# A product with two weights side by side, and the place of the scores of wide tiles

## The reference

```python
for t in range(S):                                   # S = 768, heads of D = 40
    y[:, :, t] = np.einsum('bhd,bhde->bhe', rt, state)
    Sa = np.einsum('bhde,bhe->bhd', state, at)
    state_decay = state * wt[:, :, None, :] - np.einsum('bhd,bhe->bhde', Sa, bt)
    state = state_decay + np.einsum('bhd,bhe->bhde', vt, kt)
...
h = np.maximum(x @ w_in, 0.0)                        # 320 -> 1024
conv_out += conv_w[k][None, None, :] * hp[:, k:k + S, :]
return (h * gate @ w_out).astype(np.float32)
...
for e in range(E):                                   # E = 4, Hd = 64
    scores = scale * (q @ k.transpose(0, 2, 1))
    scores = np.where(causal, -1000000000.0, scores)
    scores = scores - scores.max(-1, keepdims=True)
    a = np.exp(scores)
    a /= a.sum(-1, keepdims=True) + 1e-09
    ye = a @ v @ wo[e]
```

## Time and profile before

| | us |
|---|---|
| three runs | 920.96, 911.47, 918.24 (median 918.24) |
| the profiled execution | 923.58 |
| its span, first to last instruction | 921.9 |
| PE busy | 824.6 (89%), 11,872 matmuls |
| weight loads | 597.0 (65%) |
| DVE busy | 559.7 (61%) |
| ACT busy | 317.4 (34%) |
| POOL busy | 259.5 (28%) |
| mean granted clock of PE | 0.946 |

### The profile page before, as it was taken

One profiled execution on the slowest core, in us unless ns is written; L12 is line 12 of the kernel. 1 busy time (PEld: TensorE's weight loads), 2 busy tenths in 40 slices (PEclk: granted clock), 3 DMA queues, 4 the chain that ended last, 5 costly groups with the idle time before them and its releaser, 6 DMA issues.

```text
span 921.9 us, 27713 instructions
## 1 busy us (share of the span) xinstructions
PE 824.6 (89%) x11872; PEld 597.0 (65%) x11872; DVE 559.7 (61%) x1235; ACT 317.4 (34%) x741; POOL 259.5 (28%) x525
## 2 busy tenths in 40 slices
PE   3428989998999988889998999988999998999988
PEld 3428889988998988864465654545644656545555
DVE  8995795878599742136528645357464277354474
ACT  4102331323133232222227542246432266322364
POOL 2087777778778877000000000000000000000000
PEclk9999895979599798899999999999999979999999
DMA  3645575657566574620100000100001000000000
GB/s 117 153 85 122 126 163 113 134 139 140 122 157 138 113 158 102 157 78 26 44 1 15 16 15 1 43 0 23 15 8 43 1 8 22 16 1 0 1 15 30
DMA packets 130922, 61.33 MB, mean 67 GB/s; under 512 B 106544, under 2 KB 119792, under 8 KB 130800
## 3 DMA queue, kind: packets, MB, share of 16 engines
q1 hardware_dynamic: 96156, 32.61, 16.3%
q10 hardware_dynamic: 34644, 26.95, 11.3%
HBM read 45.37 MB, written 14.16 MB: 65 GB/s over the span
## 4 chain that ended last, share of the span: by engine, by line
PE 75%; DVE 11%; issue 5%; ACT 5%; POOL 2%; DMA 1%; SPq 0%; ACTq 0%; DVEq 0%
PE ps_all L808 8%; PE ps_all L792 8%; PE ps_scan L105 5%; PE ps_all L852 5%; PE ps_scan L188 4%; PE ps_all L918 4%; PE ps_all L900 4%; PE ps_all L930 4%; PE ps_scan L130 3%; PE ps_scan L167 3%; PE ps_all L795 3%; PE ps_all L802 2%; PE ps_all L835 2%; PE ps_scan L122 2%; PE ps_scan L114 2%
## 5 line engine op out<-in xcount | busy, mean ns | idle before, releaser
L328 POOL TENSOR_TENSOR t_update<-solver_then_w_down 128x133 f32<-128x133 f32 (+13 forms) x251 | 118.6, 473 | 88.1 <-DMA solver_then_w_down<-l_blocks 39.1
L330 POOL TENSOR_TENSOR solver_then_w_down<-solver_then_w_down,t_update 128x133 f32<-128x133 f32 (+13 forms) x251 | 132.7, 529 | 19.7
L105 PE MATMUL ps_scan<-decayed_a_and_eye,scaled_then_x 40*128 40x104 f32 x768 | 67.6, 345 | 46.5 <-DVE decayed_a_and_eye L362 45.2
L1129 DVE TENSOR_REDUCE minus_max<-ps_all 128x1 f32<-128x128 f32 (+5 forms) x96 | 55.3, 617 | 66.8 <-PE ps_all L904 66.8
L105 PEld LDWEIGHTS ps_scan<-decayed_a_and_eye,scaled_then_x 40*128 40x128 f32 x768 | 62.8, 252 | 48.6 <-issue 47.7
L808 PE MATMUL ps_all<-gated,solver_then_w_down 128*128 128x384 f32 x256 | 91.1, 499 | 0.0
L792 PE MATMUL ps_all<-scaled_then_x,inputs_then_w_up 128*128 128x384 f32 x256 | 88.8, 490 | 1.8 <-ACT ak_l_then_ffn L970 1.8
L1028 ACT ACTIVATE probs_t<-ps_all 128x512 f32<-128x512 f32 (+3 forms) x128 | 55.1, 452 | 69.9 <-PE ps_all L918 69.3
L808 PEld LDWEIGHTS ps_all<-gated,solver_then_w_down 128*128 128x128 f32 x256 | 46.0, 189 | 44.6 <-issue 19.1
L792 PEld LDWEIGHTS ps_all<-scaled_then_x,inputs_then_w_up 128*128 128x128 f32 x256 | 47.6, 190 | 36.3 <-ACT ak_l_then_ffn L970 6.0
L232 ACT ACTIVATE x_rhs<-ps_scan 128x320 f32<-128x320 f32 x48 | 21.0, 438 | 141.3 <-PE ps_scan L122 70.5
(11 more groups left out here) (117 smaller groups left out, 1523.8 us busy)
## 6 DMA issues: line engine op xcount, KB each, us to landing
r_t_and_v_t<-in_rv ACTq DMA_DIRECT2D x48, 160.0 KB
inputs_then_w_up<-in_x ACTq DMA_DIRECT2D x46, 160.0 KB
solver_then_w_down<-l_blocks SPq DMA_DIRECT2D x22, 256.0 KB, 4.6
uv_and_ruv<-in_v ACTq DMA_DIRECT2D x48, 80.0 KB, 3.7
y_t<-y_out SPq DMA_DIRECT2D x24, 160.0 KB
out<-out_rows SPq DMA_DIRECT2D x24, 160.0 KB, 1.8
inputs_then_w_up<-in_x ACTq DMA_DIRECT2D x46, 81.4 KB
inputs_then_w_up<-in_x ACTq DMA_DIRECT2D x46, 80.0 KB
```

The costliest lines, as they stand in the source:

```text
L105: last = nc.tensor.matmul(PS[:, o:o + ROWS], weights, AL[c % NK][rows(h), p, :], start=True, stop=True)
L328: return (lambda: eng.tensor_tensor(tmp[:, 0:cols, 0:rest], l[:, s:s + 1, s + 1:BLK].broadcast_to(shape), t[:, 0:cols, s:s + 1].broadcast_ ...
L330: lambda: eng.tensor_tensor(t[:, 0:cols, s + 1:BLK], t[:, 0:cols, s + 1:BLK], tmp[:, 0:cols, 0:rest], ALU.subtract))
L1129: nc.vector.tensor_reduce(NM[:, v:v + 1], PS[:, first_bank(v) * 512:first_bank(v) * 512 + n], AX.X, ALU.min).then_inc(m["nm"], 1)
```

## The change

Two edits.

First, the tiles of r, v and u become one, `v_t_u_t_r_t` (`VUR`, three buffers): for each position p three pieces of 64 columns. For head 0 they are v, u, r, for head 1 they are r, u, v, so that v and u (or u and v) stand side by side and make one weight operand of 40 x 128. `uv_r` then has one product for each p and h, 16 in all, that writes all 128 partitions of `PH[h]`. ACT copies u into the middle piece, and `u_t` goes. The DRAM input has the same three pieces, the middle one zero, and the DMA loads all three.

```diff
-    RV = [sb(f"r_t_and_v_t{n}", [ROWS, 2, P8, C]) for n in range(3)]
-    RT = [RV[n][:, 0, :, :] for n in range(3)]
-    VT = [RV[n][:, 1, :, :] for n in range(3)]
+    VUR = [sb(f"v_t_u_t_r_t{n}", [ROWS, P8, 3, C]) for n in range(3)]
+    RT = lambda n, h: VUR[n][rows(h), :, 2 - 2 * h, :]
+    UT = [VUR[n][:, :, 1, :] for n in range(3)]
...
                 for h in range(2):
-                    nc.tensor.matmul(PH[h][own(h), seg(p, C)], VT[n % 3][rows(h), p, :], RT[n % 3][rows(h), p, :],
-                                     start=True, stop=True)
-                for h in range(2):
-                    last = nc.tensor.matmul(PH[h][own(1 - h), seg(p, C)], UT[rows(h), p, :], RT[n % 3][rows(h), p, :],
+                    last = nc.tensor.matmul(PH[h][:, seg(p, C)], VUR[n % 3][rows(h), p, h:h + 2, :].rearrange("r k t -> r (k t)"), RT(n % 3, h)[:, p, :],
                                             start=True, stop=True)
...
-                act.dma_start(RV[n % 3][rows(h), :, :, :].rearrange("r k p t -> r (k p t)"),
-                              in_rv[n, h].rearrange("r k p t -> r (k p t)")).then_inc(m[f"r{n % 3}"], 16)
+                act.dma_start(VUR[n % 3][rows(h), :, :, :].rearrange("r p k t -> r (p k t)"),
+                              in_rv[n, h].rearrange("r p k t -> r (p k t)")).then_inc(m[f"r{n % 3}"], 16)
...
-                nc.scalar.activation(UT[:, :, :], by8(PU, C)[0:ROWS], ACT.Copy, scale=-1.0).then_inc(m["ut_sb"], 1)
+                nc.scalar.activation(UT[n % 3], by8(PU, C)[0:ROWS], ACT.Copy, scale=-1.0).then_inc(m["ut_sb"], 1)
```

Second, in PE's loop over pairs, `scores(w)` of a wide pair moves behind the transposes of unit 2(w-2) and `values(w-3)`:

```diff
         for w in range(NW + LAG_O - 1):
-            if w < NW:
+            wide = 2 * w >= WIDE
+            if w < NW and not wide:
                 scores(w)
             if 0 <= w - LAG_T < NW:
                 transposes(2 * (w - LAG_T))
             if 0 <= w - LAG_PV < NW:
                 values(w - LAG_PV)
+            if w < NW and wide:
+                scores(w)
             if 0 <= w - LAG_T < NW:
                 transposes(2 * (w - LAG_T) + 1)
```

More of the change, by code:

```diff
@@ L61, in recurrence @@
     ZS = sb("x_rhs2", [128, P8, D])
-    UT = sb("u_t", [ROWS, P8, C])
     ST = [sb(f"state{x}", [ROWS, P8, D]) for x in range(NPAR)]
@@ L176, in out_from_state @@
                     o = place(6, p) + D
-                    nc.tensor.matmul(PS[rows(h), o:o + C], STT[n % 2][rows(h), p, :], RT[n % 3][rows(h), p, :],
+                    nc.tensor.matmul(PS[rows(h), o:o + C], STT[n % 2][rows(h), p, :], RT(n % 3, h)[:, p, :],
                                      start=(p % 4 == 0), stop=False, skip_group_check=True)
```

6 lines of the change are left out of this document (5 added, 1 removed).

## The result

The changed kernel took **986.92 us** as a median of four runs (982.8 to 994.74), the kernel before 919.6 us beside it (911.47 to 922.18): ratio 1.076 (1.066 to 1.086). Slower was right, but the time lies 31 us above the forecast of 956 and outside its range of 938 to 976. The profiled execution took 988.72 us, 65.1 more than that of before; its recurrence ends 31.5 us later (435.7 instead of 404.2), and what comes behind it takes 33.6 us more, 8.4 for each of the four batches.

The account below looks back on a forecast made before the run. PE was taken to bound the recurrence, and a loop over other engines the wide attention pairs. Change 1 (+18 us) and change 2 (+20) made +38: 961.6 us profiled, 956 us as a median, range 938 to 976.

Parts of the forecast that it names:

- What bounds the kernel: Recurrence bound by PE, 28% of the time at the low clock; wide attention pairs by a loop over DVE and ACT.
- Change 1, the block: uv_r in the recurrence: weight loads set the pace, 2.0 us high and 3.7 low against 1.0 and 1.9; +27.5 us.
- Change 1, the holes: Ten PE waits for "issue" before x_from_state (L122) in the recurrence vanish, with matmul tails: -8.9 us.
- Change 1, the clock: Recurrence: low share kept as before, 4.4 of 24 steps low; no added cost in the sum.
- Layout, loads and the strided copy: Recurrence: loads growing from 160 to 240 KB and u's copy in 8 pieces are hidden; priced at nothing.
- Change 2: Attention, pairs 8 to 11: scores behind transposes and values join a longer loop over DVE; 5 us a batch, +20 us.
- upper bound: Attention: PE's idle stretches of 1 to 2.5 us also bring a low-clock window, some 3 us more a batch.
- hidden weights: Rival, uv_r: only streaming counts, the block stays at 1.0 us and the holes close; 929 us, chance 0.07.
- the instruction count: Rival, uv_r: instruction count alone sets the pace, the block takes 0.5 us; 917 us, no change, chance 0.02.
- the fit into the wait: Rival, attention: transposes and values fit into the wait for exponentials, scores(9) starting by 507.9; 926 us, chance 0.05.
- both at once: Rival: uv_r's weights hidden and transposes and values fitting into the wait; -19 us, 899 us, chance 0.03.
- the clock rival: Two more low-clock stretches in the recurrence or one in every attention: +12 to +20 us, 968 to 976, chance 0.13.

Follow-up runs that it names:

- e1: Kernel before with only the new v, u, r layout and uv_r in 16 products, attention order unchanged; 941.59 us, 26.8 over before.
- e11: The edits of e3 and e7 in one kernel; median of four runs 928.48 us, ratio 1.010 to before; fastest run 912.95 us, ratio 0.994.
- e3: e1 with each of uv_r's 16 products streaming r twice, 128 columns, the second 64 never read; 918.91 us, 22.7 less than e1.
- e4: Kernel before with the new tile, its 240 KB loads and strided copy of u, but uv_r in 32 products; 925.23 us, ratio 1.012.
- e6: Kernel before with only the values of three pairs earlier ahead of the wide scores, transposes behind; 957.87 us, 41.3 over before, ratio 1.047.
- e9: e6 with DVE's copy of o_t moved ahead of the maxima for wide pairs; 934.58 us, ratio 1.020 to the kernel before.
- e2: Kernel before with only the wide pairs' order changed: scores of pairs 8 to 11 behind transposes and values; 956.19 us, 41.4 over before.
- e8: Kernel before with the 32 products of uv_r issued twice over; 983.38 us, ratio 1.075.
- e7: Kernel before with x_from_v, x_from_state, first_blocks and all_blocks streaming 64 columns instead of 40, the extra 24 unread; 914.61 us, ratio 0.999.

## Why the prediction was wrong, step by step

The forecast added 38 us, the change cost 67.3. The step that failed is the clock, which the sum put at nothing in both parts; the holes and the waits of part 2 were mis-sized.

**What bounds the kernel.** Right: the recurrence by PE, the wide pairs by a loop over other engines. It did not ask what keeps the clock up, and this is where it failed.

**Change 1, the block: right.** Priced at 2.0 us high and 3.7 low against 1.0 and 1.9, +27.5 in all. Measured 1.93 us high; low it is 91.30 - 87.69 = 3.61 in e1. e11 has one with 128 columns streamed wholly at the low level, 3.71 us from its start to the next one by PE's timeline:

```profile
226.95 3.78 PE L160 MATMUL ps_scan<-v_t_u_t_r_t 40*128 40x128 f32 x32 [2.53 <-issue]
230.66 0.58 PE L125 MATMUL ps_scan<-state,decayed_a_and_eye 40*64 40x64 f32 x6
```

The rest of the recurrence grew by 18.6 us in the changed kernel and 20.7 in e1, with the low time taken out; 23 blocks of 0.93 us more are 21. The Trainium skill, "TensorE: Matmul & The Clock Gate", section "LDWEIGHTS (loading the stationary operand)", by which the prediction had estimated 1.7 us at either level, is not borne out for the low one.

**Change 1, the holes: right in kind, too small.** Priced at -8.9 us (6.7 and ten times 0.2 are 8.7). They went from 18.8 to 1.0 us, -17.8, in the changed kernel and to 7.3, -11.5, in e1. The step that failed is the row it was read from: L122, where the holes of the same cause before L148 and L195 (7.3 and 6.7 us) went as well. "L122's wait near nothing" is confirmed.

**Change 1, the clock: the missing term.** The prediction kept the low share as it was and named more low stretches as a rival with 0.13. In the profiled pair the low time grew from 88.7 to 157.0 us, 0.45 x 68.3 = +30.7. With block and holes: 18.6 - 17.8 + 30.7 - 2.4 (waits) = +29 us over 23 steps, forecast +17. At the high clock a step is 12.3 us (forecast 12.6); the steps of 16.9 us are the loss. e3 shows that more streaming at the same weights takes the loss of the clock away. The rival's size (12 to 20 us) is that of part 1 alone in e1, some 20, and less than the 30.7 of the changed kernel's profiled execution; it was counted as two more stretches, when the new block brings one behind 18 of 24 blocks in the changed kernel and 10 of 24 in e1.

**Layout, loads and the strided copy: priced at nothing.** e4 gives them 0.5 to 1.9% by its interval, lower clock included. By e4 the price of nothing was too low, and how much of that is chance is not settled.

**Change 2: right in mechanism, too small in size.** The walk of the first batch, from the scores of pair 7:

```
                       before   forecast   after
pair 7 to scores(8)      7.1      +1.1      +1.3
scores(8) to (9)         4.9      +1.2      +1.9
scores(9) to (10)        5.1      +1.0      +2.0
scores(10) to (11)       4.9      +2.1      +3.8
scores(11) to `up`       8.2      -0.5      -0.1
sum                               +4.9      +8.9
```

The loop was the one named, DVE's maxima, weighs and the copy of `o_t` (e6, e9). Its pieces at the high clock were right: 1.70 us from scores to maxima, and 6.9 us for a round in e6 where the last of the walk was 7.0. Missing are the low stretches: 3.4 us behind 541.3 and behind 554.9, values and scores at 1.82 and 2.26 us for 1.09 and 1.35, then 2.16 for 1.31. The prediction had them as the upper bound, "a window at the low clock, some 3 us more a batch", and took the lower value. Also missing is ACT: "some tenths" for its copies behind the second exponential were up to 1.7 us at a time, 13.8 us in the run. Four batches: 33.6 us instead of 20. How much of that is the clock can be estimated from two executions with this order: e2 has 28 us more low time behind its recurrence than the changed kernel and takes 8.3 us more there, 0.3 for each. By that, the changed kernel's 24 us more than before are worth 7 us, half of what was missed. What a stand of PE does to the clock is not tested by itself: behind the recurrence 10 us are low in e9, as before, 31 in e6 with stands of up to 2.6 us, and 62 in e2 with none over 1.9.

**Sum.** 18 + 20 became 31.5 + 33.6 in the profiled executions, and 27 + 41 by the runs of the parts alone. The rivals of hidden weights (929), of the instruction count (917), of the fit into the wait (926) and of both at once (899) are out: the block is 1.93 us, and scores(9) started 6.8 us behind scores(8), not 4.9. By kind the clock rival was nearest, but it too was too small, since it was held to strike in the recurrence or in the attention, and it struck in both.

## What to carry to other kernels

TensorE's mean clock was 0.908 in one of these kernels and 0.971 in another. So price an edit twice: by its own time, and by what it does to the clock of the work around it. The block that loads 128 columns of weights to stream 64 cost 18.6 us itself and 30.7 by the clock in the changed kernel; e3 was 23 us faster than e1 with more columns and the same loads. A stand of some 2 us was followed by 3.4 us at the low clock, in which values and scores took 1.6 us more. And before putting one piece of work ahead of another, ask what the last piece of the waited-for iteration itself waits for: here the values waited for a copy behind maxima that needed the scores which the values held up.

## What the runs showed of the hardware

- TensorE counted as busy without a pause (9.00 of 9.00 us) can run at 0.50 of its clock, and in the recurrence the falls came 2.2 to 3.5 us behind the start of the block with side by side weights in 28 of 28 cases (changed kernel and e1).
- Streaming 64 or 128 columns against the same 128 columns of weights takes the same time to 3% (1.93 and 1.99 us a block), and the block doubles at the low clock (3.61 and 3.71 us).
- TensorE can outrun its instructions: 64 more short matmuls a step, with their weight loads, took the waits for "issue" from 26.2 to 51.5 us, and 32 fewer took them to 8.6. All 51 holes over 0.15 us in the recurrences of before and e8 end 2.2 to 3.0 us behind the start of a packet of the code queue.
- None of the twelve kernels was shown to be faster than the one before; e7 is at 0.999, and e11, with one run of 912.95 us, has no interval.
